# Two FFNs after pooled attention on one core: when the first gated form of pair 1 is split, and in which order GpSimd makes its column sums

## The chip, the cores and the metric

The kernel runs on one core of a Trainium2 chip. The metric is the device time of one launch in microseconds; of several executions the median counts.

## The reference

```python
attn = softmax(q @ pool8(k).T / sqrt(D)) @ pool8(v)          # B, H, S, D = 4, 8, 576, 64
x = attn as [2304 tokens, 512]
xn = x / sqrt(mean(x * x) + 1e-6) * rms_g
y = (silu(xn @ w_gate) * (xn @ w_val)) @ w_out                # first FFN, 512 -> 1536 -> 512
out = silu(y @ w2_in) @ w2_out                                # second FFN, 512 -> 2048 -> 512
```

All in float32.

## The kernel before

**Tiling.** The 2304 tokens are three pairs of two blocks of 384. After the attention the kernel goes through six phases: first FFN of pair 0 (phase 0), first FFN of pair 1 (phase 1), second FFN of pair 0 (2), first FFN of pair 2 (3), second FFN of pair 1 (4) and of pair 2 (5). An FFN's up projection is cut into units of 256 columns. In a first FFN a group is two units, G (gate) and V (value); phase 1 holds units 12 to 23, so unit 20 is G of group 4, unit 21 V of group 4, units 22 and 23 G and V of group 5. Unit 24 is the first of phase 2.

**Seven products.** Every product is done in Strassen's way, with seven products of sums ("forms") in place of eight, and every float32 operand is split into a rounded high part and the low rest, so that each is three matmuls (L1993 to L1995 in a unit). A unit has 7 x 6 = 42 matmuls. ScalarE copies the first product out of its bank (`keep_first`, L1175), VectorE adds the second product to that copy (`combine_u2`, L1564) and then the fourth and fifth (`combine_u3`, L1572 and L1575), then the last two (L1583). TensorE's fourth product goes into the bank of the second and waits for `combine_u2`; its sixth waits for the first half of `combine_u3`. In a G unit ScalarE takes the silu of the four blocks (two of them while the next unit has begun); in a V unit VectorE multiplies them with the values (`gate`, L1598).

**The whole product.** In phases 1 and 3 (WHOLES) the down projection isn't done group by group: the gated blocks of all six groups stay in `hid`, and after the last unit one large product over the full depth follows (`whole`, L2089 to L2091), again seven forms, each 2 x 18 = 36 matmuls. Before each form, its hidden side is split in PART = 3 parts: ScalarE makes the high parts (`form_high`, L1245, into `fh`), VectorE the low ones (`form_low`, L1625, into `fl`). The first form (f = 0) needs only groups 0 to 2. The others are column sums of hid: GpSimd makes those of form two (f = 3, L964) and of form four (f = 5, L968) in `hidden_sums`, each in three parts; VectorE makes f = 4 and f = 6 (L1632). A sum f = 3 writes over the block that the first form reads, and so waits for its low part; a sum f = 5 needs the gated blocks of groups 3 to 5, the last of which is ready with unit 23's last gate. Form four's matmuls also wait for a bank sum of form three (`whole_sum` "u2", L1649).

**Weights.** The sums and splits of the weights are made once. GpSimd makes the sums (`weight_sums`, L869 to L875) and low parts (`ring_low`, L883 to L891), ScalarE the high parts (`weight_high`, L1113 to L1119, the third of which waits for GpSimd's sums), in the slot of the ring of three that the unit will read; SyncE stores them for later phases. The weights of unit 24 go into the slot of unit 21 and wait for its products. The units of phase 1 read weights that phase 0 stored (`load_ring`, L630), a unit's load being issued when the unit three before it is done. The sums for `w_out` (six `fold_sums`, L907 to L917) are stored by SyncE as `fold_home`; their buffer shares its place with parts of `fh`, and so the first `form_high` waits for the last store.

**Order.** Each engine has its own list of instructions, written out by a loop over the same items (units, downs, wholes, endings); across engines only semaphores order them. An engine does its list strictly in order, so a waiting instruction holds all behind it.

Of the kernel before, what the change touches and what calls it, by code (L numbers as in the profile page):

```python
# [20 lines left out]
def ffn_kernel(nc, q, k, v, w_gate, w_val, w_out, rms_g, w2_in, w2_out, out):  # L21
# [265 lines left out]
    with ctx:  # L287
# [502 lines left out]
        def _(pool):  # L790
# [165 lines left out]
            def hidden_sums(e, f, j):  # L956


                b11, b12, b21, b22 = [hid[e][:, i, 2 * j:2 * j + 2, :] for i in range(4)]
                first_group = downs.index((WHOLES[e], 0))  # L960
                if f == 3:
                    pool.wait_ge(s_flo, PART * NF * e + j + 1)
                    pool.wait_ge(s_hd, hd0[first_group + j + 1])
                    pool.tensor_tensor(b11, b12, b11, ALU.subtract).then_inc(s_ft, 1)  # L964
                else:
                    pool.wait_ge(s_ft, 2 * PART * e + j + 1)
                    pool.wait_ge(s_hd, hd0[first_group + PART + j + 1])
                    pool.tensor_tensor(b12, b22, b12, ALU.subtract).then_inc(s_ft, 1)  # L968
# [70 lines left out]
                    ring_low(made_at["r", 1], (1,))  # L1039

            ring_low(made_at["r", 1], (2,))
            def whole_sums(e):
                for f in (3, 5):
                    for j in range(PART):
                        hidden_sums(e, f, j)

            for i in range(2, MADE):
                if made[i][0] == "r":
                    weight_sums(i)
                    ring_low(i)  # L1050
                elif made[i][0] == "o":
                    out_low(i)
                else:
                    fold_sums(i)
                if made[i] == ("r", U2):
                    whole_sums(0)

            for j in range(CEARLY):
                ending_weight_sums(made_at["c", j])
            whole_sums(1)  # L1060
            pool.wait_ge(s_wh, 4 * NF)
            for j in range(CEARLY, 2 * EPART):
                ending_weight_sums(made_at["c", j])
# [6 lines left out]
        def _(act):  # L1070
# [141 lines left out]
            def copy_down(n):  # L1212

                ph, p = downs[n][0], pair_of[n]
                act.wait_ge(s_xlo, NF * (ph + 1))
                if ffn_of[n] == 1:
                    for i, (kind, m) in enumerate(DOWN1):
                        if kind == "perm":
                            act.wait_ge(s_down, down0[n] + i + 1)
                            act.activation(block_of(p, m, 0), ps[:, BP + m, 0:BLOCK], ACT.Copy).then_inc(s_perm, 1)  # L1220
                else:
                    for j in range(2, PT):
                        act.wait_ge(s_down, down0[n] + j + 1)
                        act.activation(tokens_of(p, j), ps[:, BP + j - 2, :], ACT.Copy).then_inc(s_perm, 1)
# [88 lines left out]
            def act_unit(x):  # L1313
                ph, letter, g, n = units[x]
                prior = ffn_of[n - 1] if n and letter != "V" and classic[n - 1] else None
                if before["unit", x] and before["unit", x][0] == "unit" and units[before["unit", x][1]][1] != "V":
                    y = before["unit", x][1]
                    for i in (2, 3):
                        silu(y, i)
                        if units[y][1] == "I" and classic[units[y][3]]:  # L1320
                            high(units[y][3], i)
                if prior == 2 and before["unit", x][0] == "down":
                    high(n - 1, 2)
                    high(n - 1, 3)
                if x == 0:
                    norm(NT - 2)
                    squares(NT - 1)

                    act.activation(idle[:, :], half[:, :], ACT.Silu)
                    norm(NT - 1)  # L1330
                    weight_high(made_at["r", 2], (0, 1))
                else:
                    keep_first(x)
                if x == 1:
                    weight_high(made_at["r", 2], (2,))
                if prior == 1:
                    high(n - 1, 1)
                    high(n - 1, 2)
                    high(n - 1, 3)
                prev = before["unit", x]  # L1340
                if prev and prev[0] == "down" and prev[1] in last_down:
                    copy_down(prev[1])
                if x == 1:
                    weight_high(made_at["o", 0])
                if x == 2:
                    weight_high(made_at["r", 3])
                if ph == 0 and letter == "V" and 1 <= g < GROUPS[1] - 1:
                    weight_high(made_at["r", x + 2])
                if ph == 0 and letter == "V" and g >= 1:
                    weight_high(made_at["o", g])  # L1350
                if x in (U2 - 2, U2 - 1):
                    weight_high(made_at["r", U2], ((0, 1), (2,))[x - U2 + 2])
                if ph == 2 and ("r", x + 1) in made_at and x > U2:
                    weight_high(made_at["r", x + 1])
                if ph == 2:
                    weight_high(made_at["o", N2 + g])
                if letter == "V" and classic[n]:
                    high(n, 0)
                elif letter != "V":
                    for i in (0, 1):  # L1360
                        silu(x, i)
                        if classic[n] and before["unit", x] and before["unit", x][0] == "whole":
                            high(n, i)
                if ph in WHOLES and (letter, g) == ("G", (PART + 1, PART)[WHOLES.index(ph)]):
                    form_high(WHOLES.index(ph), 0)
                if ph in ENDINGS and g - EPART in (1, 2):
                    ending_high(ENDINGS.index(ph), 0, ((0, 1), (2, 3))[g - EPART - 1])
                if ph in ENDINGS and x == last_unit[ph]:
                    ending_high(ENDINGS.index(ph), 1, range(EPART - 1))
# [78 lines left out]
        def _(dve):  # L1448
# [118 lines left out]
            def combine_u3(u):  # L1567
                n = units[u][3]
                if units[u][1] != "V" and n and ffn_of[n - 1] == 1:
                    dve.wait_ge(s_hd, hd0[n])  # L1570
                dve.wait_ge(s_prod, NF * u + 4)
                dve.tensor_tensor(tiles(u)[:, C22, :], ps[:, BY, 0:BLOCK], tiles(u)[:, C21, :], ALU.add)\  # L1572
                   .then_inc(s_c, 1)
                dve.wait_ge(s_c, 5 * u + 2)
                dve.tensor_tensor(tiles(u)[:, C22, :], ps[:, BZ, 0:BLOCK], tiles(u)[:, C22, :], ALU.add)\  # L1575
                   .then_inc(s_c, 1)
# [174 lines left out]
            def dve_unit(x):  # L1751
                ph, letter, g, n = units[x]
                prior = ffn_of[n - 1] if n and letter != "V" else None
                if prior == 2 and classic[n - 1] and before["unit", x][0] == "unit":
                    low(n - 1, 1)
                if prior == 2 and classic[n - 1]:
                    low(n - 1, 2)
                    low(n - 1, 3)
                if x:
                    combine_u2(x)  # L1760
                else:
                    token_part(0, 4 + XORDER[-1])
                if prior == 1 and before["unit", x][0] != "whole":
                    gate(x - 1, 3)
                combine_u3(x)
                if x == 0:
                    scale_x(NT - 2)
                if prior == 1 and classic[n - 1]:
                    low(n - 1, 1)
                    low(n - 1, 2)  # L1770
                    low(n - 1, 3)
                if letter == "V":
                    gate(x, 0)
                combine_last(x, C21)
                if classic[n] and before["unit", x] and before["unit", x][0] == "whole":
                    low(n, 0)
                if letter == "V":
                    gate(x, 1)
                combine_last(x, C12)
                if letter == "V":  # L1780
                    gate(x, 2)
                    if classic[n]:
                        low(n, 0)
                if ph in WHOLES:
                    e = WHOLES.index(ph)
                    form_low(e, 0, ({9: (0,), 10: (1, 2)}, {7: (0,), 8: (1,), 9: (2,)})[e].get(x - first_unit[ph], ()))
                if ph in ENDINGS and g - EPART in (1, 2):
                    ending_low(ENDINGS.index(ph), 0, ((0, 1), (2, 3))[g - EPART - 1])

# [398 lines left out]
```

## Time and profile before

| | us |
|---|---|
| median of 3 runs | 870.52 (869.14 to 872.47) |
| the profiled execution | 869.81 |
| its span, first to last instruction | 868.1 |
| TensorE busy in it | 852.5 (98%) |
| VectorE / GpSimd / ScalarE busy | 554.8 / 423.6 / 359.5 |

The table is one execution. TensorE is busy nearly throughout, so time can be read as TensorE's waits, found in the list of who waited for whom, and placed with the timeline. Matmul rows overlap: a row's start and the next row's start give the pace.

### The profile page before, as it was taken

The numbers are of one execution on the slowest core, as the hardware profiler recorded it, in microseconds if no ns is written. First come the engines' busy times: TensorE is split into PE (matmuls) and PEld (weight loads), VectorE is DVE, ScalarE is ACT, GpSimd is POOL, SyncE is SP. The second block draws the span as 40 slices with busy tenths as digits, with TensorE's granted clock in tenths as the row PEclk, the third lists the DMA queues.
The fourth block names the chain that finished last, engine by engine and source line by source line (L and its number), as shares of the span: only waits on it lengthen the run. The fifth ranks groups of instructions, "written<-read, shape, count | busy, mean of one in ns | idle before, by whom it ended". The sixth has DMA issues, their size and how long they took to land.

```text
span 868.1 us, 13900 instructions
## 1 busy us (share of the span) xinstructions
PE 852.5 (98%) x5292; PEld 831.6 (96%) x5292; DVE 554.8 (64%) x835; ACT 359.5 (41%) x640; POOL 423.6 (49%) x415
## 2 busy tenths in 40 slices
PE   7999999999999898999999999999999999999998
PEld 6999999999999898999989899999999999999998
DVE  6689757776546469966564435569734788335873
ACT  3689745442221225545544221315433444134521
POOL 6898999883528354477874035270061700003400
PEclk9999999999999999999999999999999999999999
DMA  9971678778869967567579579997779757687762
GB/s 257 277 207 37 230 273 322 273 301 307 330 223 406 412 236 252 202 230 293 200 286 388 186 267 352 359 408 282 276 266 362 271 195 279 243 330 247 257 233 110
DMA packets 94801, 235.78 MB, mean 272 GB/s; under 512 B 23056, under 2 KB 69136, under 8 KB 83216
## 3 DMA queue, kind: packets, MB, share of 16 engines
q1 hardware_dynamic: 94736, 234.90, 75.0%
q8 instruction: 42, 0.69, 0.3%
q14 instruction: 23, 0.19, 0.1%
HBM read 164.10 MB, written 70.78 MB: 271 GB/s over the span
## 4 chain that ended last, share of the span: by engine, by line
PE 61%; DVE 1%; issue 1%; ACT 0%; DVEq 0%
PE ps L1993 10%; PE ps L1995 10%; PE ps L1994 10%; PE ps L2131 5%; PE ps L2130 5%; PE ps L2129 5%; PE ps L2089 3%; PE ps L2090 3%; PE ps L2091 3%; PE ps L2060 3%; PE ps L2061 3%; PE ps L2059 3%; DVE hid L1632 0%; DVE fl L1625 0%; ACT fh L1245 0%
## 5 line engine op out<-in xcount | busy, mean ns | idle before, releaser
L1993 PE MATMUL ps<-xh,wr 128*128 128x384 f32 x840 | 283.6, 338 | 3.2 <-DVE vt L1564 2.9
L1995 PE MATMUL ps<-xh,wr 128*128 128x384 f32 x840 | 281.8, 336 | 0.0
L1994 PE MATMUL ps<-xl,wr 128*128 128x384 f32 x840 | 281.6, 335 | 0.0
L1993 PEld LDWEIGHTS ps<-xh,wr 128*128 128x128 f32 x840 | 158.2, 188 | 7.1 <-DVE vt L1564 3.3
L1994 PEld LDWEIGHTS ps<-xl,wr 128*128 128x128 f32 x840 | 158.2, 188 | 0.3
L1995 PEld LDWEIGHTS ps<-xh,wr 128*128 128x128 f32 x840 | 158.1, 188 | 0.0
L2131 PE MATMUL ps<-ew,efl 128*128 128x256 f32 x336 | 95.1, 283 | 0.0
L2129 PE MATMUL ps<-ew,efh 128*128 128x256 f32 x336 | 95.1, 283 | 0.0
L2130 PE MATMUL ps<-ew,efh 128*128 128x256 f32 x336 | 95.1, 283 | 0.0
L1583 DVE TENSOR_TENSOR qt<-ps,qt 128x384 f32<-128x384 f32 x84 | 46.2, 555 | 49.8 <-PE ps L1995 49.8
L950 POOL TENSOR_TENSOR eh<-eh 128x768 f32<-128x768 f32 x8 | 17.2, 2167 | 122.6 <-DVE efl L1660 122.6
L2130 PEld LDWEIGHTS ps<-ew,efh 128*128 128x128 f32 x336 | 64.5, 192 | 0.0
L2131 PEld LDWEIGHTS ps<-ew,efl 128*128 128x128 f32 x336 | 64.5, 192 | 0.0
L2129 PEld LDWEIGHTS ps<-ew,efh 128*128 128x128 f32 x336 | 64.5, 192 | 0.0
L1175 ACT ACTIVATE qt<-ps 128x384 f32<-128x384 f32 x42 | 20.7, 492 | 105.0 <-PE ps L1995 104.6
L1660 DVE TENSOR_TENSOR efl<-eh,efh 128x768 fp32r<-128x768 f32 x56 | 59.8, 1123 | 5.0 <-ACT efh L1275 5.0
L930 POOL TENSOR_TENSOR ebt<-raw_z 128x256 f32<-128x256 f32 x8 | 5.9, 738 | 112.0 <-PE ps L2091 40.0
L1275 ACT ACTIVATE efh<-eh 128x768 fp32r<-128x768 f32 x56 | 43.0, 835 | 41.2 <-PE ps L2131 41.2
L2089 PE MATMUL ps<-fh,fw 128*128 128x384 f32 x168 | 56.4, 336 | 2.7 <-DVE fl L1625 1.8
L2091 PE MATMUL ps<-fh,fw 128*128 128x384 f32 x168 | 56.2, 334 | 0.0
L2090 PE MATMUL ps<-fl,fw 128*128 128x384 f32 x168 | 56.2, 334 | 0.0
L1572 DVE TENSOR_TENSOR qt<-ps,qt 128x384 f32<-128x384 f32 x42 | 23.4, 557 | 50.9 <-PE ps L1995 50.8
(198 smaller groups left out, 1772.4 us busy)
## 6 DMA issues: line engine op xcount, KB each, us to landing
wr<-ring_home SPq DMA_DIRECT2D x40, 1792.0 KB, 9.6
ring_home<-wr SPq DMA_DIRECT2D x20, 1792.0 KB, 8.0
ew<-ending_home SPq DMA_DIRECT2D x8, 2048.0 KB, 8.7
out_home<-wo SPq DMA_DIRECT2D x14, 1024.0 KB, 9.6
fw<-fold_home SPq DMA_DIRECT2D x8, 1536.0 KB, 7.2
ew<-out_home SPq DMA_DIRECT2D x24, 512.0 KB, 7.1
fw<-out_home SPq DMA_DIRECT2D x18, 512.0 KB, 6.7
ending_home<-eb SPq DMA_DIRECT2D x16, 512.0 KB, 10.7
```

What stands on the lines that cost most here:

```text
L1275: act.activation(efh[e][i % 2][:, 2 * j:2 * j + 2, :], ending_part(f, j), ACT.Copy).then_inc(s_ehi, 1)
L1583: dve.tensor_tensor(done if units[u][1] == "V" else qt[:, c, :], done, tiles(u)[:, c, :], ALU.add)\
L1660: dve.tensor_tensor(efl[e][i % 2][:, 2 * j:2 * j + 2, :], ending_part(f, j), efh[e][i % 2][:, 2 * j:2 * j + 2, :], ALU.subtract).then_inc( ...
L1993: pe.matmul(out_ps, w_hi, x_hi, start=first and c == 0, stop=False, skip_group_check=True)
L1994: pe.matmul(out_ps, w_hi, x_lo, start=False, stop=False, skip_group_check=True)
L1995: ins = pe.matmul(out_ps, w_lo, x_hi, start=False, stop=c == 1, skip_group_check=True)
L2089: pe.matmul(out_ps, w_hi, h_hi, start=first and c == 0, stop=False, skip_group_check=True)
L2090: pe.matmul(out_ps, w_hi, h_lo, start=False, stop=False, skip_group_check=True)
L2091: ins = pe.matmul(out_ps, w_lo, h_hi, start=False, stop=c == 2 * PART - 1, skip_group_check=True)
L2129: pe.matmul(out_ps, h_hi, w_hi, start=first and c == 0, stop=False, skip_group_check=True)
L2130: pe.matmul(out_ps, h_hi, w_lo, start=False, stop=False, skip_group_check=True)
L2131: ins = pe.matmul(out_ps, h_lo, w_hi, start=False, stop=c == 2 * EPART - 1, skip_group_check=True)
```

## The change

In pair 1's first FFN (phase 1, e = 0) three lists are reordered. No instruction is added or removed.

- ScalarE: the three high parts of the first form stood at the end of unit 20's work, ahead of that unit's last two silus and of unit 21's bank copy. Now they follow unit 21's bank copy. The high parts of unit 24's weights, which were divided over units 22 (first two) and 23 (third), are all in unit 22.
- VectorE: the first low part stood at the end of unit 21, the second and third at the end of unit 22. Now the first lies in unit 21 between `combine_u2` and `combine_u3`, the second at the end of unit 21, the third at the end of unit 22.
- GpSimd: the six column sums followed the sums and low parts of unit 24's weights. Now the first comes ahead of them, the second after two thirds of the low parts, the third and the three of f = 5 after the rest.

Pair 2's first FFN (e = 1) stays as it was.

```diff
             ring_low(made_at["r", 1], (2,))
-            def whole_sums(e):
-                for f in (3, 5):
+            for i in range(2, MADE):
+                if made[i] == ("r", U2):
+                    hidden_sums(0, 3, 0)
+                    weight_sums(i)
+                    ring_low(i, (0, 1))
+                    hidden_sums(0, 3, 1)
+                    ring_low(i, (2,))
+                    hidden_sums(0, 3, 2)
                     for j in range(PART):
-                        hidden_sums(e, f, j)
-
-            for i in range(2, MADE):
-                if made[i][0] == "r":
+                        hidden_sums(0, 5, j)
+                elif made[i][0] == "r":
                     weight_sums(i)
                     ring_low(i)
...
-                if made[i] == ("r", U2):
-                    whole_sums(0)
...
-            whole_sums(1)
+            for f in (3, 5):
+                for j in range(PART):
+                    hidden_sums(1, f, j)
...
+                if ph == WHOLES[0] and x == last_unit[ph] - 2:
+                    form_high(0, 0)
...
-                if x in (U2 - 2, U2 - 1):
-                    weight_high(made_at["r", U2], ((0, 1), (2,))[x - U2 + 2])
+                if x == U2 - 2:
+                    weight_high(made_at["r", U2])
...
-                if ph in WHOLES and (letter, g) == ("G", (PART + 1, PART)[WHOLES.index(ph)]):
-                    form_high(WHOLES.index(ph), 0)
+                if ph == WHOLES[1] and (letter, g) == ("G", PART):
+                    form_high(1, 0)
...
+                if ph == WHOLES[0] and x == last_unit[ph] - 2:
+                    form_low(0, 0, (0,))
                 combine_u3(x)
...
-                    form_low(e, 0, ({9: (0,), 10: (1, 2)}, {7: (0,), 8: (1,), 9: (2,)})[e].get(x - first_unit[ph], ()))
+                    form_low(e, 0, ({9: (1,), 10: (2,)}, {7: (0,), 8: (1,), 9: (2,)})[e].get(x - first_unit[ph], ()))
```

## Rows read from the trace of the kernel before

**Rows 1.** The page's busy times: us, share of the span, instructions
```profile
PE 852.5 (98%) x5292; PEld 831.6 (96%) x5292; DVE 554.8 (64%) x835; ACT 359.5 (41%) x640; POOL 423.6 (49%) x415
```
**Rows 2.** TensorE's waits, whole run: total us, times, longest
```profile
PE ps L1993 <- DVE vt L1564: 2.9, 1, 2.9
PE ps L2089 <- DVE fl L1625: 1.8, 2, 1.1
...
PE ps L2089 <- issue: 0.9, 1, 0.9
```
**Rows 3.** TensorE's timeline, 300 to 346 us: start, us, instruction [idle before, releaser]
```profile
300.16 0.34 PE L1995 MATMUL ps<-xh,wr 128*128 128x384 f32 x1
303.35 0.69 PE L1993 MATMUL ps<-xh,wr 128*128 128x384 f32 x1 [2.85 <-DVE vt L1564]
...
306.58 0.34 PE L1994 MATMUL ps<-xl,wr 128*128 128x384 f32 x1
...
323.65 0.33 PE L2089 MATMUL ps<-fh,fw 128*128 128x384 f32 x1
...
331.80 0.34 PE L2091 MATMUL ps<-fh,fw 128*128 128x384 f32 x1
...
333.22 0.44 PE L2089 MATMUL ps<-fh,fw 128*128 128x384 f32 x1 [1.08 <-DVE fl L1625]
...
338.42 0.41 PE L2089 MATMUL ps<-fh,fw 128*128 128x384 f32 x1 [0.75 <-DVE fl L1625]
...
345.79 0.41 PE L2089 MATMUL ps<-fh,fw 128*128 128x384 f32 x1 [0.89 <-issue]
```
**Rows 4.** Busy us by stretch; behind the engines the granted clock
```profile
303.35:306.40 3.05, 3.05 (x10) 3.05 (x10) 0.69 (x2) 0.00 (x0) 0.00 (x0) 0.50 0.98 391
```
**Rows 5.** ScalarE's timeline, 299 to 318 us
```profile
299.10 2.31 ACT L1245 ACTIVATE fh<-hid 128x768 fp32r<-128x768 f32 x3 [2.89 <-DMA fold_home<-fb]
...
302.14 0.47 ACT L1175 ACTIVATE vt<-ps 128x384 f32<-128x384 f32 x1
...
314.41 0.49 ACT L1188 ACTIVATE qt<-ps 128x384 f32<-128x384 f32 x1 [2.85 <-PE ps L1995]
...
317.92 1.05 ACT L1119 ACTIVATE wr<-wt 128x1024 fp32r<-128x1024 f32 x1
```
**Rows 6.** VectorE's timeline, 316 to 346 us; the second low part also alone
```profile
316.97 1.81 DVE L1625 TENSOR_TENSOR fl<-hid,fh 128x768 fp32r<-128x768 f32 x2
...
326.52 6.64 DVE L1625 TENSOR_TENSOR fl<-hid,fh 128x768 fp32r<-128x768 f32 x3 [0.92 <-ACT fh L1245]
...
328.06 2.59 DVE L1625 TENSOR_TENSOR fl<-hid,fh 128x768 fp32r<-128x768 f32 x1
...
333.09 4.32 DVE L1632 TENSOR_TENSOR hid<-hid 128x768 f32<-128x768 f32 x3
...
345.15 0.54 DVE L1649 TENSOR_TENSOR xacc<-ps,xacc 128x384 f32<-128x384 f32 x1
```
**Rows 7.** GpSimd's timeline, 314 to 335 us
```profile
314.32 0.74 POOL L887 TENSOR_TENSOR wr<-raw_c,wr 128x256 fp32r<-128x256 f32 x1
319.05 1.29 POOL L890 TENSOR_TENSOR wr<-wt,wr 128x512 fp32r<-128x512 f32 x1 [3.99 <-ACT wr L1119]
...
321.54 5.77 POOL L964 TENSOR_TENSOR hid<-hid 128x768 f32<-128x768 f32 x3
327.28 7.57 POOL L968 TENSOR_TENSOR hid<-hid 128x768 f32<-128x768 f32 x3
```
**Rows 8.** VectorE's timeline at the start of pair 2's whole product
```profile
586.60 3.63 DVE L1625 TENSOR_TENSOR fl<-hid,fh 128x768 fp32r<-128x768 f32 x3 [0.91 <-ACT fh L1245]
590.15 2.68 DVE L1632 TENSOR_TENSOR hid<-hid 128x768 f32<-128x768 f32 x3
```
**Rows 9.** The load of unit 22's weights: its issue, then KB and us to landing
```profile
291.71 1.28 SPq L630 DMA_DIRECT2D wr<-ring_home  x1
...
wr<-ring_home SPq DMA_DIRECT2D x1, 1792.0 KB, 11.5
```

## The prediction

> **What bounds the kernel now.** I read the page's table of engines first. TensorE is busy 852.5 of 868.1 us [rows 1]: only a wait of TensorE, or a stretch at a lower clock, can give time back. Next the list of TensorE's waits over the whole run. Its three largest all lie near the change [rows 2]: 2.9 us on VectorE's sum into vt, 1.8 us in two waits on VectorE's low parts (fl), and 0.9 us that the list calls "issue". Last, the timeline of TensorE between 300 and 346 us, since a wait costs more than its listed length [rows 3].
>
> The measure is the spacing of undisturbed matmuls: from 323.65 to 331.80 us there are 47 steps, so 0.1734 us each.
>
> First stretch: the matmul at 300.16 is followed by one at 303.35 us, and the eleventh step after 300.16 starts at 306.58. Eleven steps should take 1.91 us and took 6.42: 4.51 us lost. Of this 3.02 us is the wait, and 1.50 us is the ten steps behind it, spaced 0.323 us. In that stretch the granted clock was 0.50, which is the 1.2 GHz level [rows 4]. The clock fell while TensorE stood idle, so it belongs to the wait and goes with it.
>
> Second stretch: the whole product of pair 1 starts at 323.65 us and its fourth form at 345.79. Between lie 3 x 36 = 108 matmuls, 18.73 us at full spacing; they took 22.14. Lost: 3.41 us, split by the rows after each wait as 1.25 (third part of form two, 333.22 instead of 331.97), 1.04 (form three, 338.42 instead of 337.38) and 1.13 (form four, 345.79 instead of 344.66).
>
> Together 7.92 us. Why each is there:
>
> - ScalarE stood 2.89 us waiting for the store of the last fold weights before the first high part, at 299.10 us. It had two silus and the bank copy of unit 21 queued behind its three high parts: the copy came at 302.14 [rows 5], VectorE's sum into vt followed it, and TensorE's fourth product followed that. Unit 21 had begun 18 steps before 300.33, at 297.21, so its first product was done at about 298.4 and the copy was 3.7 us late.
> - In the whole product GpSimd's six column sums run from 321.54 to 334.85 us [rows 7]. VectorE's low parts lie beside them and take up to 2.59 us each instead of 0.9 (1.81 for the two at 316.97) [rows 6]; its three sums of hid, 4.32 us where the same three take 2.68 in pair 2 [rows 6, 8]. The lateness ends in fl (two waits) and, behind VectorE's queue, in the bank sum at 345.15 us, 0.64 us ahead of TensorE's restart. That is the wait called "issue": form four waits for this bank sum.
>
> **The change part by part.** Times "new" are those of before less 4.5 us once unit 21 has not stalled.
>
> *High parts behind the copy.* The silus of unit 20 run at about 296.9 and 298.0 (their sums end then), the copy at 298.4 to 298.9. The store was out by 299.1, where the wait for it ended [rows 5]. So the three high parts run 299.1 to 301.4 with nothing of ScalarE's behind them until the next unit's copy, a unit (42 x 0.1734 = 7.3 us) later. VectorE's sum into vt can then run when product two is done, 299.5 to 300.1, and TensorE goes on at 300.33. Gain 4.51 us, clock included.
>
> *First low part between VectorE's two combinations in unit 21.* Its high part is ready at 299.95. It takes 300.1 to 301.0. The combination behind it needs product four, done at 297.21 + 24 x 0.1734 + 0.16 = 301.5. Cost nothing; 0.5 us of cover. TensorE needs the first result of that combination (0.56 us long) at product six, 302.4: 0.8 us of lateness in all is free, after that each microsecond is one of TensorE. The second low part comes in unit 21's tail, the third in unit 22's: there one instruction instead of two, 1.81 down to about 0.9 us [rows 6].
>
> *GpSimd.* The first column sum starts at 301.0 and ends at 302.9. The sums for unit 24's weights wait for unit 21's products, 304.5: 1.6 us of cover. They and two thirds of the low parts end as before, 315.06 less 4.5 = 310.5 [rows 7]. Then column sum two to 312.4, the rest of the low weights (two of 1.29 us, row at 319.05 [rows 7]) to about 315, column sum three to 317, and two of the (0,5) sums to about 321. One is left for the last gate at 321.1. Six sums that ended 11.2 us after the whole product's start now end 4 us after it.
>
> *Whole product.* Pair 2 is this arrangement, seen in the same trace: only its last column sum meets VectorE's low parts, which take 3.63 us for three, the three hid sums 2.68 [rows 8]; none of TensorE's listed waits lies in its whole product. In new times: low parts of form two 322.0 to 325.6, needed from 325.4 (third part 327.5); hid sums to 328.3; low part one of form three at 329.2, needed 331.6; four VectorE items later the bank sum ends about 337.0, needed 337.9. All three waits go: 3.41 us. The thinnest cover is that bank sum's 0.9 us.
>
> *Third part of the weights' high copy, now in unit 22.* ScalarE waits there for GpSimd's sums, 308.6 new, and copies 1.05 us [rows 5] to 309.7. The silu behind it came at 314.41, new 309.9 [rows 5]. Cost nothing; TensorE needs this silu at unit 23's start, 311.9, so 1.4 us more is free. The earlier finish also lets SyncE store unit 24's weights earlier; behind that store in its queue are the fold loads, none of them due before.
>
> *A new meeting.* The third low part on VectorE starts at 312.5 (316.97 less 4.5), when GpSimd has just begun the rest of the low weights. The rows price a low part beside GpSimd between 0.9 (no harm) and 2.59 us [rows 6]. I take 1.29 of waiting and 0.9 of work, about 2.1 us, the nearest GpSimd row being 1.29 long; it ends at 314.5. The bank combination behind it then ends at 315.05, against TensorE's need at 311.85 + 18 steps = 314.97. Before, it had to follow two low parts that ended at 318.78, with 0.1 us of cover (unit 23's fourth product was due at 323.65 - 24 x 0.1734 = 319.49, and it takes 0.56 us) [rows 3, 6]. Cost 0.2 us; bounds 0 and 0.7.
> By the Trainium skill, SBUF — State Buffer, "SBUF: two separate sides", the port pair that GpSimd shares with VectorE is locked for a whole instruction when VectorE has two SBUF inputs, and the loser blocks. That rule speaks against putting GpSimd work beside any low part. The trace agrees: 2.59 us is near to 0.9 plus a column sum of 1.9. By it the sum has the 0.2 above; without it, 0.
>
> *Sum.* 4.51 + 3.41 - 0.2 = 7.7 us. The profiled execution took 869.8 us (span 868.1 and 1.7 around it), so 862.1. That execution is 0.7 under the median of 870.5: against the median 862.8 us.
>
> **Rivals.**
> 1. *The chain of column sums slips.* GpSimd's queue now waits for VectorE's second and third low parts. If it slips until two or more sums again meet VectorE's form-two low parts, up to 3.4 us stays: 866.2. For it: each sum is 1.9 us (5.77 for three) [rows 7] and the queue has no gap from 304.5 to 321. Against: pair 2 needs only that one sum remain. 0.13, at 864 to 866.2.
> 2. *A transfer ends the first stretch.* Unit 22's weights were issued at 291.71 and took 11.5 us, to 303.2 [rows 9]. Unit 22 now starts at 304.5, not 309.0: cover 1.3 us.  A flight 3 us longer costs 1.7 us, 864.5. A store of fold weights 1 to 3 us late costs up to 2 us by the 0.8 above. 0.12, at 864 to 866.
> 3. *Nothing moves:* the three high parts were not what delayed the copy, or the new low part takes their place in full. The 2.89 us on the store just ahead of them speaks against. 0.04, 870.5.
> 4. *The other side: slower.* The same load of unit 22, much later: a stall L there drops the clock too and costs L + 1.5 (by the first stretch). It decides from L = 6.2 us on, a flight of 19.0 us where the row has 11.5; at 24 us the kernel takes 876. Nothing but the load would have to change. 0.03.
>
> **How the numbers follow.** The forecast has 0.68: 862.8, its own range 861.3 to 864.2 (the 0 to 0.7 of the meeting, and some 1 us by which the median of three runs can lie off, from 869.1 to 872.5 before). Rivals 1 and 2 lie above, 864 to 866.2; the range takes in most of them and leaves out rivals 3 and 4 and a little of both ends: 861.2 to 865.8. Half a per cent, about what a measurement of this kernel can tell from no change, is 4.35 us: faster means under 866.2. That holds for the forecast and nearly all of rivals 1 and 2: 0.88. Within: 0.09. Slower: 0.03.
>
> **What would show it.** In the profile after: TensorE's waits hold neither vt (L1564's counterpart) nor fl, the "issue" of 0.9 is gone, and what remains is at most 0.2 to 0.7 us in unit 23's fourth product. The mean granted clock is 1.00 in every stretch near 300 us. ScalarE's copy of unit 21 stands at about 298.4, ahead of three high parts at 299.1. GpSimd's last column sum starts within 0.5 us of the last gate. VectorE's first three low parts of form two take 3.6 us, not 6.64. I am wrong if TensorE waits in unit 21's sixth product (store late), at unit 22's start (weights late), or again in forms two to four.

## The result, and the profile after

| | before | after |
|---|---|---|
| median, us | 870.56 (869.14 to 872.47) | 862.30 (861.26 to 862.47) |
| profiled execution / span | 869.81 / 868.1 | 862.45 / 860.7 |

The ratio is 0.9901 (95% interval 0.9881 to 0.9922), 8.3 us by the medians. One later execution of the kernel before took 927.8 us at a mean clock of 0.851, and it is left out of every number here.

TensorE's waits from 285 us to the end, where [rows 2] has three, are an empty list in the kernel after. Its timeline (start, us, instruction; idle time before it would stand in brackets) answers to [rows 3]:

```profile
300.23 0.34 PE L2003 MATMUL ps<-xh,wr 128*128 128x384 f32 x1
300.40 0.38 PE L2001 MATMUL ps<-xh,wr 128*128 128x384 f32 x1
...
315.10 0.44 PE L2001 MATMUL ps<-xh,wr 128*128 128x384 f32 x1
315.38 0.34 PE L2002 MATMUL ps<-xl,wr 128*128 128x384 f32 x1
...
319.39 0.33 PE L2097 MATMUL ps<-fh,fw 128*128 128x384 f32 x1
...
338.12 0.33 PE L2097 MATMUL ps<-fh,fw 128*128 128x384 f32 x1
```

The fourth product of unit 21 starts at 300.40, right behind the third; it had stood until 303.35. From the whole product's first matmul (319.39) to its fourth form (338.12) are 18.73 us, 108 steps of 0.1734, where 22.14 had passed. What is left of a stall is one step of 0.28 instead of 0.17 us at 315.10, in unit 23's fourth product. From 289.2 us on (a matmul at 289.21 before and at 289.27 after) the fourth form is reached 7.73 us sooner. The busy times by stretch, with the granted clock behind the engines, answer to [rows 4]:

```profile
300.50:304.00 3.50, 3.50 (x22) 3.50 (x22) 2.48 (x5) 1.07 (x2) 1.84 (x1) 1.00 0.97 410
```

ScalarE's timeline after, where [rows 5] stood:

```profile
298.52 0.49 ACT L1179 ACTIVATE vt<-ps 128x384 f32<-128x384 f32 x1
299.25 2.32 ACT L1249 ACTIVATE fh<-hid 128x768 fp32r<-128x768 f32 x3 [0.24 <-DMA fold_home<-fb]
...
308.77 1.06 ACT L1123 ACTIVATE wr<-wt 128x1024 fp32r<-128x1024 f32 x1 [1.58 <-POOL wt L875]
310.07 0.49 ACT L1192 ACTIVATE qt<-ps 128x384 f32<-128x384 f32 x1 [0.23 <-PE ps L2003]
```

The bank copy is 3.6 us earlier, and the wait for the store has fallen from 2.89 to 0.24 us because the copy now fills that time. The weights' third high part is at 308.77, not 317.92, and costs the silu behind it nothing. VectorE's timeline after, for [rows 6]:

```profile
300.20 0.95 DVE L1631 TENSOR_TENSOR fl<-hid,fh 128x768 fp32r<-128x768 f32 x1
...
312.65 1.93 DVE L1631 TENSOR_TENSOR fl<-hid,fh 128x768 fp32r<-128x768 f32 x1
314.50 0.54 DVE L1570 TENSOR_TENSOR vt<-ps,vt 128x384 f32<-128x384 f32 x1
...
322.48 3.64 DVE L1631 TENSOR_TENSOR fl<-hid,fh 128x768 fp32r<-128x768 f32 x3 [0.92 <-ACT fh L1249]
326.04 2.68 DVE L1638 TENSOR_TENSOR hid<-hid 128x768 f32<-128x768 f32 x3
...
336.46 0.54 DVE L1655 TENSOR_TENSOR xacc<-ps,xacc 128x384 f32<-128x384 f32 x1
```

Three low parts of form two take 3.64 us, not 6.64, the hid sums 2.68, not 4.32: the figures of pair 2 [rows 8] to within 0.01 us. The low part at 312.65 takes 1.93 us beside GpSimd. GpSimd's column sums after, for [rows 7]:

```profile
315.69 1.84 POOL L964 TENSOR_TENSOR hid<-hid 128x768 f32<-128x768 f32 x1
317.50 3.65 POOL L968 TENSOR_TENSOR hid<-hid 128x768 f32<-128x768 f32 x2
321.70 1.85 POOL L968 TENSOR_TENSOR hid<-hid 128x768 f32<-128x768 f32 x1 [0.56 <-DVE hid L1604]
```

They end at 323.55, 4.2 us after the whole product's start; before it was 11.2 us. By the profile the prediction stands. The experiments ask which edit earned what.

### The profile page after: what moved, and what is told of

Read it like the earlier page. It is cut to its first block, busy times and chain, and to the rows that moved or that the text cites. A ratio compares the mean times of both kernels' runs of the same rounds, so it can differ in the third digit from the quotient of the medians.

```text
span 860.7 us, 13899 instructions
## 1 busy us (share of the span) xinstructions
PE 850.8 (99%) x5292; PEld 830.6 (96%) x5292; DVE 551.4 (64%) x835; ACT 360.0 (42%) x640; POOL 421.2 (49%) x415
## 4 chain that ended last, share of the span: by engine, by line
PE 96%; DMA 2%; POOL 1%; DVE 0%; SPq 0%; issue 0%; DVEq 0%; POOLq 0%
PE ps L2001 17%; PE ps L2003 17%; PE ps L2002 17%; PE ps L2139 5%; PE ps L2138 5%; PE ps L2137 5%; PE ps L2099 3%; PE ps L2097 3%; PE ps L2098 3%; PE ps L1931 3%; PE ps L2068 3%; PE ps L2069 3%; PE ps L2067 3%; PE ps L2044 2%; PE ps L2043 2%; PE ps L2042 2%
```

## The experiments

Each ratio is against the kernel before, run on the same chip.

**High parts behind the copy, alone** (the kernel before with this on ScalarE; VectorE, GpSimd and the weights' high parts as before):

```diff
+                if ph == WHOLES[0] and x == last_unit[ph] - 2:
+                    form_high(0, 0)
...
-                if ph in WHOLES and (letter, g) == ("G", (PART + 1, PART)[WHOLES.index(ph)]):
-                    form_high(WHOLES.index(ph), 0)
+                if ph == WHOLES[1] and (letter, g) == ("G", PART):
+                    form_high(1, 0)
```

> Only ScalarE's list changes: the three high parts behind unit 21's bank copy. My theory, two losses that do not depend on each other: unit 21's wait and its stretch at the lower clock go (4.5 us), the whole product keeps its 3.4 us: 866.0 us, ratio 0.9948. Rival, the second loss follows from the first (a kernel that is 4.5 us late there has all its engines late in the same way, but the early high parts start the chain of low parts sooner): part of the 3.4 goes too, 863 to 865. Rival, the low part had to move with the high parts: 868 or more.

865.26 us, ratio 0.9952 (0.9934 to 0.9971). Its list of TensorE's waits from 285 us on:

```profile
PE ps L2091 <- DVE fl L1627: 1.9, 2, 1.1
PE ps L2091 <- issue: 0.9, 1, 0.9
```

Unit 21's wait is gone whole, the whole product's three waits stay whole: from its first matmul to form four it takes 22.18 us, before 22.14. The two losses are separate, and the rivals fall.

**GpSimd's order, alone** (the kernel before with the new list of GpSimd).

> Only GpSimd's list changes; its first column sum must wait for a low part that VectorE makes only at 310.4 to 311.5 us. My theory: the 4.5 us of unit 21 stay, and the six sums, though 2 us late in the queue, end some 4 us sooner than before, so 2.9 to 3.4 us of the whole product's loss go: 867.1 to 867.6, ratio 0.9961 to 0.9967. Rival, this order is worth nothing without the early low part, because the sums for unit 24's weights start late: 869 to 871.

869.30 us, ratio 1.0001 (0.9986 to 1.0015): nothing gained by the medians, against my 2.9 to 3.4 us. VectorE's timeline in the profiled execution (867.3 us, the quickest of ten):

```profile
314.94 2.76 DVE L1629 TENSOR_TENSOR fl<-hid,fh 128x768 fp32r<-128x768 f32 x2
...
323.92 2.00 DVE L1602 TENSOR_TENSOR hid<-qt,vt 128x384 f32<-128x384 f32 x1
326.84 4.99 DVE L1629 TENSOR_TENSOR fl<-hid,fh 128x768 fp32r<-128x768 f32 x3 [0.92 <-ACT fh L1249]
```

And TensorE's:

```profile
318.22 0.44 PE L1997 MATMUL ps<-xh,wr 128*128 128x384 f32 x1 [0.67 <-DVE vt L1568]
...
322.51 0.33 PE L2093 MATMUL ps<-fh,fw 128*128 128x384 f32 x1
...
331.01 0.44 PE L2093 MATMUL ps<-fh,fw 128*128 128x384 f32 x1 [1.05 <-DVE fl L1629]
...
342.82 0.41 PE L2093 MATMUL ps<-fh,fw 128*128 128x384 f32 x1
```

The first column sum waited for the late first low part and pushed the weights' sums back, as the rival had it. Of the three waits in the whole product one of 1.05 us was left, but a new one of 0.67 us came in unit 23: the two low parts at unit 22's end now met GpSimd's work (2.76 us, before 1.81). The whole product up to form four still takes 20.31 us (322.51 to 342.82), 1.6 more than at full pace: here the last gate met a column sum too (2.00 us; 0.76 in the kernel after), and the low parts of form two began late. So something was gained, and lost again in part. The three executions at a mean clock of 1.000 have a median of 867.5 us, where those of the kernel before on this chip have 868.2: 0.7 us gained. Two of the ten show a mean of 0.996, which none of the kernel before on this chip does, and the medians hide the gain.

**The changed kernel with GpSimd's old order.**

> The changed kernel with GpSimd's six column sums back behind unit 24's weights. My theory: the whole product's three waits come back whole, 3.4 us less the 0.1 us of the meeting in unit 23: 862.3 + 3.3 = 865.6, ratio 0.9943, with VectorE's first three low parts of form two at about 6.6 us. Rival, the low parts' new places had already opened the second stretch: 862.3 to 863.5.

862.54 us, ratio 0.9918 (0.9898 to 0.9939). My theory failed: nearly all of the second stretch's gain stays without the interleaving. VectorE, GpSimd and TensorE in this kernel:

```profile
322.50 5.00 DVE L1627 TENSOR_TENSOR fl<-hid,fh 128x768 fp32r<-128x768 f32 x3 [0.91 <-ACT fh L1245]
```
```profile
310.70 1.31 POOL L890 TENSOR_TENSOR wr<-wt,wr 128x512 fp32r<-128x512 f32 x1
...
319.33 6.49 POOL L968 TENSOR_TENSOR hid<-hid 128x768 f32<-128x768 f32 x3
```
```profile
319.36 0.33 PE L2093 MATMUL ps<-fh,fw 128*128 128x384 f32 x1
...
338.50 0.41 PE L2093 MATMUL ps<-fh,fw 128*128 128x384 f32 x1
```

The weights' last low parts start at 310.70, where with the high parts alone they stood at 315.09 waiting for ScalarE's third high part of the weights. So the sums start 4.4 us earlier through an edit on ScalarE that I had costed at nothing. Two of them still meet the low parts of form two (5.00 us for three), and that costs TensorE little: from 319.36 to 338.50 are 19.14 us, 0.41 more than after the full change, most of it in a restart at 338.50 that is 0.26 us late.

**The weights' third high part in unit 22, alone** (the kernel before with this):

```diff
-                if x in (U2 - 2, U2 - 1):
-                    weight_high(made_at["r", U2], ((0, 1), (2,))[x - U2 + 2])
+                if x == U2 - 2:
+                    weight_high(made_at["r", U2])
```

> The kernel before with one edit: the third high part of unit 24's weights in unit 22 instead of 23. My theory now: this edit, which I had costed at nothing, ends GpSimd's low parts 4.4 us earlier, starts the six column sums 4.4 us earlier and takes 3.0 to 3.4 us of the whole product's loss; unit 21's wait stays: 3 us under the kernel before, ratio 0.9965. Rival: early low parts on VectorE are needed for it as well: no change against before.

868.58 us, ratio 0.9990 (0.9979 to 1.0002): 0.7 us by the medians, not the 3 I expected. TensorE's timeline:

```profile
321.37 0.44 PE L1993 MATMUL ps<-xh,wr 128*128 128x384 f32 x1 [1.79 <-DVE vt L1564]
```

No wait is left in its whole product, but there is this one of 1.79 us in unit 23, and in the profiled execution a second stretch at the lower clock behind it. The next run shows the same without unit 21's wait.

**Both edits of ScalarE** (the first and the last diff), VectorE and GpSimd as before.

> ScalarE's two edits together (high parts behind the copy, the weights' third high part in unit 22), VectorE and GpSimd as before. My theory now: all of the gain but 0.2 to 0.4 us: 862.3 to 862.9, ratio 0.992 or a little under, TensorE without a wait of over 0.4 us in the whole product. Rival, VectorE's new places carry a part of it: 863.5 to 865.

864.63 us, ratio 0.9946 (0.9930 to 0.9963): the rival. VectorE's timeline, then TensorE's, then two stretches with their granted clocks:

```profile
312.39 3.88 DVE L1627 TENSOR_TENSOR fl<-hid,fh 128x768 fp32r<-128x768 f32 x2
...
325.50 3.63 DVE L1627 TENSOR_TENSOR fl<-hid,fh 128x768 fp32r<-128x768 f32 x3 [0.91 <-ACT fh L1245]
```
```profile
314.66 0.34 PE L1997 MATMUL ps<-xh,wr 128*128 128x384 f32 x1
316.79 0.44 PE L1995 MATMUL ps<-xh,wr 128*128 128x384 f32 x1 [1.79 <-DVE vt L1566]
```
```profile
316.79:318.10 1.31, 1.31 (x7) 1.31 (x8) 0.00 (x0) 0.00 (x0) 1.31 (x2) 1.00 0.95 225
318.11:321.31 3.20, 3.20 (x12) 3.20 (x12) 1.67 (x3) 0.00 (x0) 3.20 (x2) 0.50 0.96 409
```

The whole product is as quick as after the full change, but GpSimd's sums now start at 312.90, when VectorE makes its two low parts at the end of unit 22. They take 3.88 us instead of 1.81, the sum into vt is late, and TensorE waits 1.79 us. Moving one low part into unit 21, so that a single one stands there, is what the change on VectorE adds. This kernel and the changed one with GpSimd's old order differ in VectorE's list alone: 864.6 and 862.5 us, 2.1 between them, the clock included. The two executions here at a mean clock of 1.000 took 863.4 and 863.8, the two at 0.998 took 865.4 and 865.8.

**The changed kernel with the weights' third high part back in unit 23.**

> The changed kernel with the weights' third high part back in unit 23. Theory, the two edits are two ways to the same 3.4 us: GpSimd's interleaving alone also leaves only one or two sums beside VectorE's low parts of form two, since one sum now fills the time in which GpSimd waits for ScalarE: 862.3 to 862.8. Rival, the interleaving does nothing by itself and the 3.3 us come back: 865.3 to 865.8, as with only the high parts moved.

862.04 us, ratio 0.9918 (0.9901 to 0.9934): as the full change. VectorE's and GpSimd's timelines:

```profile
311.60 0.95 DVE L1631 TENSOR_TENSOR fl<-hid,fh 128x768 fp32r<-128x768 f32 x1
...
321.16 4.99 DVE L1631 TENSOR_TENSOR fl<-hid,fh 128x768 fp32r<-128x768 f32 x3 [0.91 <-ACT fh L1249]
```
```profile
309.62 1.84 POOL L964 TENSOR_TENSOR hid<-hid 128x768 f32<-128x768 f32 x1
313.68 1.29 POOL L890 TENSOR_TENSOR wr<-wt,wr 128x512 fp32r<-128x512 f32 x1 [2.22 <-ACT wr L1123]
```

A column sum stands in the time in which GpSimd waits for ScalarE, and the third low part meets nothing (0.95 us). The whole product takes 18.86 us up to form four, 0.13 more than after the full change. With either of interleaving and early weights the other adds nothing that these runs can tell. That the interleaving earns the 3.4 us by itself here is read from GpSimd's rows: the kernel with high parts and VectorE's moves, but neither of the two, was not run.

**The meeting itself** (only the high parts moved, and GpSimd's f = 5 sums of pair 1 cut short, with the rest of those sums left out):

```diff
+                    if e == 0:
+                        b12, b22 = b12[:, :, 0:8], b22[:, :, 0:8]
                     pool.tensor_tensor(b12, b22, b12, ALU.subtract).then_inc(s_ft, 1)
```

> Only the high parts moved (as in the run that gave 865.3), and GpSimd's three f = 5 sums of pair 1 cover 8 of 384 columns, so the rest of those sums is left out. Theory, the 3.4 us of the whole product are the meeting of GpSimd's sums with VectorE's low parts: VectorE's three low parts of form two take 3 to 4 us instead of 6.64, no wait of TensorE is left there, 862.2 to 862.6. Rival, VectorE is late because GpSimd's f = 3 sums are late: the waits stay at 2 us or more, 864.5 or more.

861.50 us, ratio 0.9911 (0.9896 to 0.9925), and no wait of TensorE from 285 us on. VectorE's and GpSimd's rows:

```profile
321.64 3.39 DVE L1629 TENSOR_TENSOR fl<-hid,fh 128x768 fp32r<-128x768 f32 x3 [0.91 <-ACT fh L1247]
324.96 2.71 DVE L1636 TENSOR_TENSOR hid<-hid 128x768 f32<-128x768 f32 x3
```
```profile
316.65 5.78 POOL L964 TENSOR_TENSOR hid<-hid 128x768 f32<-128x768 f32 x3
322.40 2.71 POOL L970 TENSOR_TENSOR hid<-hid 128x16 f32<-128x16 f32 x3
```

The order of all lists is that of the 865.3 us kernel, and the f = 3 sums are as late as there: they start 2.1 us before the whole product in both. Only the length of the f = 5 sums has changed, and the 3.4 us are gone: the second stretch was the meeting. The Trainium skill, SBUF — State Buffer, "SBUF: two separate sides", says that a VectorE instruction with two SBUF inputs and a GpSimd one that reads SBUF take the shared port pair for a whole instruction each, and that the one that comes second blocks. The runs agree: three low parts took 3.6 us beside one column sum, 5.0 beside two, 6.64 beside three.

**High parts behind the silus, ahead of the copy** (the changed kernel with `form_high(0, 0)` moved to just before `keep_first`).

> The changed kernel with the three high parts behind unit 20's silus but ahead of unit 21's bank copy. My theory: the copy is at 301.5 instead of 298.5, VectorE's sum ends at 302.6, TensorE waits 2.2 us in unit 21's fourth product. If the granted clock falls with that wait too, another 1.5 us: 866.0; if not, 864.5. Rival, it was the silus behind the high parts that held TensorE and not the copy: 862.3, nothing lost.

864.89 us, ratio 0.9948 (0.9931 to 0.9966). TensorE's timeline, and a stretch behind the wait with its granted clock:

```profile
299.23 0.34 PE L2003 MATMUL ps<-xh,wr 128*128 128x384 f32 x1
301.64 0.44 PE L2001 MATMUL ps<-xh,wr 128*128 128x384 f32 x1 [2.08 <-DVE vt L1570]
```
```profile
302.70:306.00 3.30, 3.30 (x21) 3.30 (x20) 2.45 (x5) 0.00 (x0) 1.67 (x1) 1.00 0.98 377
```

The wait follows the copy, as forecast; the silus alone had little to do with it. The clock is mixed: this execution kept 1.00 and took 863.4 us, two of the six show a mean of 0.998 and took 865.7 and 866.4. A third took 866.1 at a mean of 1.000, and that one these records don't explain.

**One high part ahead of the copy, two behind.**

> The changed kernel with the first high part ahead of unit 21's bank copy and two behind it. The copy waits for the store (299.1) and one part (0.84 us), 300.0 to 300.5, the sum ends at 301.1: TensorE waits 0.6 to 0.8 us in unit 21's fourth product, 863.0 with the clock at its full level; 1.5 us more in the executions in which it falls. Rival, a wait this short never brings the clock down: all executions within 862.6 to 863.4.

863.89 us, ratio 0.9932 (0.9909 to 0.9955), above my 863.0, with a wait of 0.60 us in the profiled execution (863.4 us). Four of five executions lie between 862.9 and 864.5; the fifth took 866.6 at a mean clock of 0.994. I have no trace of that one, so whether this short wait began it stays open.

**Lateness put in ahead of the first high part** (the changed kernel with one, and with two, additional copies there):

```diff
+                    if (e, i, j) == (0, 0, 0):
+                        for k in range(1):          # 2 in the second
+                            act.activation(fh[0][0][0][:, :, :], hidden_part(0, f, 0), ACT.Copy).then_inc(s_extra, 1)
+                            act.wait_ge(s_extra, k + 1)
```

> The changed kernel with one additional ScalarE copy of 128x768 ahead of the first high part, waited for, as if the store of the fold weights had landed 0.9 us later. By the prediction 0.8 us of lateness is free (VectorE's first combination of unit 21 would end at 302.5 instead of 302.3, due about 302.4): TensorE waits 0 to 0.2 us in unit 21's sixth product, 862.3 to 862.5. Rival, the cover is not there and each microsecond counts from the start: 863.2.

862.39 us, ratio 0.9910 (0.9882 to 0.9938), no wait. VectorE's first low part:

```profile
301.20 0.96 DVE L1636 TENSOR_TENSOR fl<-hid,fh 128x768 fp32r<-128x768 f32 x1 [0.58 <-ACT fh L1254]
```

> The same with two additional copies, 1.9 us late. By the prediction TensorE waits 1.0 to 1.1 us in unit 21's sixth product: 863.3 to 863.5 with the clock at its full level, 1.5 us more if it falls. Rival, the lateness is taken up on the way because VectorE has idle time in unit 21: 862.3.

864.02 us, ratio 0.9927 (0.9902 to 0.9953). VectorE's first low part with two, then TensorE's timeline:

```profile
302.19 0.96 DVE L1636 TENSOR_TENSOR fl<-hid,fh 128x768 fp32r<-128x768 f32 x1 [1.79 <-ACT fh L1254]
```

```profile
302.50 0.34 PE L2008 MATMUL ps<-xh,wr 128*128 128x384 f32 x1
303.68 0.45 PE L2006 MATMUL ps<-xh,wr 128*128 128x384 f32 x1 [0.84 <-DVE vt L1583]
```

Counted from unit 21's fourth product (300.40 after, 300.74 and 300.52 here), the first low part starts 0.66 us later with one copy and 1.87 us later with two. The 0.66 cost nothing; of the 1.87 TensorE pays 1.18 - 0.17 = 1.0 us. So 0.9 us was free: the cover of 0.8 us is real, and it is all there is.

## Why the prediction was right, step by step

- *Unit 21's wait and its clock, 4.51 us.* The mechanism is shown by the run with the high parts alone and by the one that puts them ahead of the copy again. The size is a mixture. In 35 executions of the kernel before, beside these experiments, 21 have a mean clock of 0.998 and a median of 870.05 us, 13 have 1.000 and 868.37, and one has 0.996. The 1.5 us behind the wait are real but, by these means, paid in some two executions of three; I had put them into every one. The profiled execution was one that paid. None of the four of the kernel after shows less than 0.999. "The clock fell while TensorE stood idle" is too strong as well: with both edits of ScalarE TensorE had been back at full pace for 1.3 us (316.79 to 318.10) before the clock fell. That the fall goes with the wait still holds.
- *The whole product, 3.41 us.* The size and the cause (VectorE's low parts beside GpSimd's sums) are right. What failed is "Third part of the weights' high copy, now in unit 22 [...] Cost nothing": it costs nothing, but I saw only its cost. Without it, or without the interleaving to which I gave the whole term, the 3.41 us still go, less 0.1 and 0.4; without both, and with VectorE's list as before, they stay. Its other effect is a price: it moves GpSimd's work under the low parts at unit 22's end.
- *First low part between the combinations: "Cost nothing".* Right, with the cover of 0.8 us as measured. But what it earns was not in the sum. It takes a low part away from unit 22's end, and without that the early weights give 1.96 us back in unit 23 (314.66 to 316.79, less one step), and 1.5 more when the clock falls.
- *The new meeting, 0.2 us.* The low part took 1.93 us (I said 2.1) and ended at 314.58 (314.5); the matmul behind it lost about 0.1 us.
- *Rival 1.* Its threshold was wrong. Two column sums beside the low parts cost 0.1 and 0.4 us, not "up to 3.4". The cover in the whole product takes nearly all of 1.4 us of VectorE's lateness (5.0 against 3.6 us) but not 4.6 (6.64, and 1.6 in the hid sums). With GpSimd's order alone the low parts were no slower (4.99), but they began 1.2 us later in the whole product than after the full change, behind the slowed gate, and together that cost 1.6 us.
- *Rival 2.* Unit 22's weights, issued at 292.86, took 10.5 us, to 303.4; unit 22 started at about 304.6. The cover was 1.3 us, as forecast, and nothing came of it.
- *Sum.* 7.7 us forecast, 7.73 in the stretch; 862.8 forecast, 862.3 measured. That both hit so closely is luck in part. The profiled execution before had paid for the clock, as the sum assumes. And the 8.3 us by the medians are at the high end: beside the experiments, with medians of 869.3 to 870.1 for the kernel before, the three kernels without a listed wait of over 0.2 us and with nothing left out (old order of GpSimd, late weights, one additional copy) gained 6.9, 7.3 and 7.7 us.

## What to carry to other kernels

When a copy that frees an accumulator bank stands in an in-order queue behind work that waits for a transfer, put the work behind the copy: here that alone gave 4.2 us. Before GpSimd's elementwise work is given a new place, list which two-input VectorE instructions it will meet there and how much lateness the next consumer bears; three meetings in one place cost 3.4 us, one or two 0 to 0.4 us, and two with a slowed gate ahead of them 1.6. An edit costed at nothing still moves what was waiting for it: ask both what it costs and whom it releases, and undo the parts of a change singly before crediting one.

## What the runs showed of the hardware

By the executions' mean clocks, a short wait of TensorE brings its clock to the lower level in some executions and not in others. In the traces, the wait of 2.85 us in [rows 3] was followed at once by a stretch at 0.50 (1.2 GHz). A wait of 1.79 us was followed by one too, 1.3 us after TensorE had gone on. One of 2.08 us left the clock at 1.00, as did one of 2.71 us in unit 21 of the run with GpSimd's order alone. So one profile can't tell what such a wait costs; the mean clocks of many executions can give a share.
